# A gated linear attention with routed experts on one core: chunks laid out by halves, one product instruction a step of the running products, and a block closed without the drain of GpSimd's queue

## What is computed

```
mag = sqrt(a_re**2 + a_im**2); scale = min(mag, 0.999) / (mag + 1e-6)
a = (a_re + i a_im) * scale                        # complex gate, per batch, head, token, dim
for t in range(S):                                 # S = 768, B = 4, H = 8, D = 48
    state = a[t][:, None] * state                  # complex
    state.re += outer(k[t], v[t])
    y[t] = q[t] @ state.re
x = y as (B*S, H*D) = (3072, 384)
e = argmax(x @ w_gate + modality_bias[modality_id]); g = its softmax weight   # 8 experts
x = g * (relu(x @ w1[e]) @ w2[e])                  # w1 384x1024, w2 1024x384
out = ((x @ mid_w1) * (x @ mid_w2)) @ w3 @ w_out
```

## Time and profile before

| what | value |
|---|---|
| time, median of 3 runs | 917.78 us (916.23 to 918.56) |
| time of the profiled execution | 917.5 us, of which its span is 915.7 us |
| PE busy | 768.6 us (84%) |
| DVE busy | 496.7 us (54%) |
| ACT busy | 331.2 us (36%) |
| POOL busy | 128.7 us (14%) |

### The profile page before, as it was taken

How to read it: one execution, slowest core, us unless ns; L and a number is a source line. 1 busy time by engine, 2 the same in 40 slices (tenths; PEclk the granted TensorE clock), 3 DMA queues, 4 the chain that set the end, 5 groups by cost and what they waited for, 6 DMA issues and landing times.

```text
span 915.7 us, 11775 instructions
## 1 busy us (share of the span) xinstructions
PE 768.6 (84%) x4541; PEld 641.9 (70%) x4541; DVE 496.7 (54%) x963; ACT 331.2 (36%) x657; POOL 128.7 (14%) x127
## 2 busy tenths in 40 slices
PE   0029910399999999899999999999999999999995
PEld 0015500188888888787888888888989898988885
DVE  4999999999899975866453454341111111212010
ACT  6932100354545434534453452333122222223120
POOL 0201100000000032410000000013232222323231
PEclk9999965599999999999999999999999999999998
DMA  9982120456666656427423430160000000000000
GB/s 380 373 270 83 69 87 0 122 147 172 185 180 165 188 161 206 141 81 238 147 96 104 128 106 9 73 207 1 35 0 35 1 26 9 18 18 9 26 1 35
DMA packets 46756, 99.19 MB, mean 108 GB/s; under 512 B 11616, under 2 KB 29920, under 8 KB 44384
## 3 DMA queue, kind: packets, MB, share of 16 engines
q1 hardware_dynamic: 41056, 79.37, 28.3%
q0 software_dynamic: 5632, 18.94, 5.9%
HBM read 60.32 MB, written 18.94 MB: 87 GB/s over the span
## 4 chain that ended last, share of the span: by engine, by line
PE 69%; DVE 19%; DMA 3%; ACT 3%; issue 2%; SPq 2%; POOL 1%; DVEq 0%
PE moe_bank L557 17%; PE moe_bank L558 17%; PE moe_bank L559 17%; PE bank L1347 4%; DVE rows L1056 3%; DVE rows L1057 3%; PE bank L1381 3%; DVE gates L1059 2%; PE bank L1397 2%; PE bank L1313 2%; DVE gates L1032 2%; DVE gates L1060 2%; DMA gates<-a_im 1%; PE bank L1401 1%; PE bank L1353 1%
## 5 line engine op out<-in xcount | busy, mean ns | idle before, releaser
L1934 DVE TENSOR_TENSOR u_sb<-x_in,moe_bank 128x512 f32<-128x512 f32 x48 | 33.0, 688 | 229.1 <-PE moe_bank L559 229.1
L1772 POOL TENSOR_TENSOR hid_lo<-u_sb,hid_hi 128x512 fp32r<-128x512 f32 x48 | 62.4, 1299 | 357.9 <-ACT hid_hi L1829 357.9
L557 PE MATMUL moe_bank<-xT_hi,w_hi 128*128 128x512 f32 x264 | 104.8, 397 | 0.0
L558 PE MATMUL moe_bank<-xT_lo,w_hi 128*128 128x512 f32 x264 | 104.8, 397 | 0.0
L559 PE MATMUL moe_bank<-xT_hi,w_lo 128*128 128x512 f32 x264 | 104.0, 394 | 0.0
L1326 PE MATMUL bank<-early_w_out,early_w3T 128*128 128x384 f32 x128 | 45.4, 512 | 66.3 <-DMA early_w_out<-w_out 62.9
L1326 PEld LDWEIGHTS bank<-early_w_out,early_w3T 128*128 128x128 f32 x128 | 24.9, 199 | 86.3 <-issue 65.0
L1848 ACT COPY x_in<-moe_bank 128x512 f32<-128x512 f32 x48 | 28.1, 586 | 143.7 <-PE moe_bank L559 143.7
L559 PE MATMUL moe_bank<-w_hi,hid_lo 128*128 128x384 f32 x192 | 64.5, 336 | 0.0
L557 PE MATMUL moe_bank<-w_hi,hid_hi 128*128 128x384 f32 x192 | 64.4, 335 | 0.0
L558 PE MATMUL moe_bank<-w_lo,hid_hi 128*128 128x384 f32 x192 | 64.4, 335 | 0.0
(11 more groups left out here) (219 smaller groups left out, 1641.1 us busy)
## 6 DMA issues: line engine op xcount, KB each, us to landing
stage<-w SPq DMA_DIRECT2D x10, 1536.0 KB, 8.3
ks<-mags SPq DMA_DIRECT2D x48, 144.0 KB, 2.8
x_sorted<-early_zero POOLq DMA_DIRECT2D x8, 772.0 KB, 21.9
qs<-gates SPq DMA_DIRECT2D x40, 146.2 KB, 2.7
gates<-a_re SPq DMA_DIRECT2D x4, 1170.0 KB, 12.3
gates<-a_im SPq DMA_DIRECT2D x4, 1170.0 KB, 14.7
x_in<-x_sorted SPq DMA_DIRECT2D x24, 193.0 KB, 3.0
spare<-k SPq DMA_DIRECT2D x4, 1152.0 KB, 5.4
```

The lines of the kernel that those rows point to most:

```text
L557: nc.tensor.matmul(out, l_hi, r_hi, start=first, stop=False)
L558: nc.tensor.matmul(out, l_hi, r_lo, start=False, stop=False)
L1772: nc.gpsimd.tensor_tensor(hid_lo[:, f], u_sb[:, f % 2], hid_hi[:, f].bitcast(F32), ALU.subtract).then_inc(u_lo_ready, 1)
L1934: nc.vector.tensor_tensor(u_sb[:, f % 2], a_sb[:, f % 2], bank_b[f % 2][:, :], ALU.mult).then_inc(u_ready, 1)
```

## The change

1. The host lays chunks out in token order, each half followed by one word of padding (pitch 65): `by_step` goes, `spaced` pads halves. All access patterns follow (`halved`, `of_halves`, `chunk_of_q`), and so do the causal mask, the token numbers, v, modality_id and the read-back in `recurrence`, in which rows of a chunk were in step order.
2. The two product instructions of a step become one of 576 elements, both inputs broadcast. The elements of token u that an instruction touches in `gates` are now 144 single words, 260 bytes apart, instead of 72 pairs.
3. In `join`, steps 0 and 1 issue one instruction each instead of two.
4. `keep_busy` issues 6 matmuls instead of 8.
5. The block is opened with `no_gpsimd_drain=True`: at its end the other four engines drain and all meet at a barrier made of semaphores alone, and POOL's own drain instruction is left out.

The core of the diff:

```diff
         prods = L.rows0[:, :, :].rearrange("p c v -> p (c v)")[:, 0:4 * NG * BLK].rearrange(
-            "p (w c n h) -> p w c n h", w=2, c=2, h=2)
+            "p (w c n) -> p w c n", w=2, c=2)
...
-            return gates[:, x, b * GB:(b + 1) * GB].rearrange("p g (c t) -> p (g c) t", t=PITCH)[:, :, 0:CH]
+            return gates[:, x, b * GB:(b + 1) * GB].rearrange("p g (r t) -> p (g r) t", t=SUB + 1)[:, :, 0:SUB]
+
+        def halved(a):
+            return a.rearrange("p c (h t) -> p (c h) t", h=2)
...
-            at = gates[:, :, :, :].rearrange("p x g (c j h) -> p x (g c) j h", j=SUB + 1, h=2)
+            at = gates[:, :, :, :].rearrange("p x g (r j) -> p x (g r) j", j=SUB + 1)
+            both = [P, 2, 2, NG * BLK]
             for u in range(SUB - 1):
-                re, im = (at[:, x:x + 1, :, u].broadcast_to([P, 2, NG * NCH, 2]) for x in (RE, IM))
                 if u:
                     dve.wait_ge(prefix_step, u)
-                nc.vector.tensor_tensor(prods[:, 0], at[:, :, :, u + 1], re, ALU.mult)
-                nc.vector.tensor_tensor(prods[:, 1], at[:, :, :, u + 1], im, ALU.mult).then_inc(products, 1)
+                nc.vector.tensor_tensor(prods, at[:, :, :, u + 1].unsqueeze(1).broadcast_to(both),
+                                        at[:, :, :, u].unsqueeze(2).broadcast_to(both), ALU.mult).then_inc(products, 1)
...
-                    last = half[:, step, :, 0, SUB - 1:SUB].broadcast_to([P, part.stop - part.start, SUB])
+                    last = half[:, step:step + 1, :, 0, SUB - 1:SUB].broadcast_to([P, 2, part.stop - part.start, SUB])
                     out = (by_re, by_im)[step]
-                    for x in (RE, IM):
-                        ins = nc.vector.tensor_tensor(out[:, x], half[:, x, :, 1, 0:SUB], last, ALU.mult)
-                    ins.then_inc(halves_done, 1)
+                    nc.vector.tensor_tensor(out, half[:, :, :, 1, 0:SUB], last, ALU.mult).then_inc(halves_done, 1)
...
+            def chunk_of_q(m, i, c):
+                return qs[m][:, i, c * PITCH:(c + 1) * PITCH].rearrange("p (h t) -> p h t", h=2)[:, :, 0:SUB]
...
-            keep_busy(8, bank_scores[0])
+            keep_busy(6, bank_scores[0])
...
-        block = ctx.enter_context(nc.Block())
+        block = ctx.enter_context(nc.Block(no_gpsimd_drain=True))
```

More of the change, by code:

```diff
@@ L48, in constants @@
     put("ident", np.eye(P))
-    when = (row % 2) * SUB + row // 2
-    put("causal", (when[:, None] <= when[None, :]) * 1.0)
+    put("causal", (row[:, None] <= row[None, :]) * 1.0)
     put("before", (row[:, None] < row[None, :]) * 1.0)
@@ L64, in constants @@
     put("region", one * (n_tiles * CH * np.arange(n_experts)))
-    put("token", when[:, None] + CH * np.arange(n_tiles)[None, :])
+    put("token", row[:, None] + CH * np.arange(n_tiles)[None, :])
     put("step", one * np.arange(n_steps))
@@ L708, in plane, with of_halves @@
         def plane(x, b):
-            return gates[:, x, b * GB:(b + 1) * GB].rearrange("p g (c t) -> p (g c) t", t=PITCH)[:, :, 0:CH]
+            return gates[:, x, b * GB:(b + 1) * GB].rearrange("p g (r t) -> p (g r) t", t=SUB + 1)[:, :, 0:SUB]
+        def halved(a):
+            return a.rearrange("p c (h t) -> p (c h) t", h=2)
+        def of_halves(part):
+            return slice(2 * part.start, 2 * part.stop)
         first_part = -(-HU * D // P) * NCH
@@ L829, in re_square @@
                 act.wait_ge(gates_in[b][RE], landed(b))
-                nc.scalar.activation(mags[b][:, :, :], plane(RE, b), ACT.Square).then_inc(re_squared, 1)
+                nc.scalar.activation(halved(mags[b][:, :, :]), plane(RE, b), ACT.Square).then_inc(re_squared, 1)
             def im_square(b):
                 act.wait_ge(gates_in[b][IM], landed(b))
-                nc.scalar.activation(squares[b], plane(IM, b), ACT.Square).then_inc(im_squared, 1)
+                nc.scalar.activation(halved(squares[b]), plane(IM, b), ACT.Square).then_inc(im_squared, 1)
             def root(b):
@@ L877, in square @@
                 out = (norms[b], seeds[b])[x]
-                nc.scalar.activation(out[:, part], plane(x, b)[:, part], ACT.Square).then_inc(p_squared, 1)
+                nc.scalar.activation(halved(out[:, part]), plane(x, b)[:, of_halves(part)], ACT.Square).then_inc(p_squared, 1)
             def log(k):
@@ L1012, in im_square @@
                 dve.wait_ge(gates_in[b][IM], landed(b))
-                nc.vector.tensor_tensor(squares[b], plane(IM, b), plane(IM, b), ALU.mult).then_inc(im_squared, 1)
+                nc.vector.tensor_tensor(halved(squares[b]), plane(IM, b), plane(IM, b), ALU.mult).then_inc(im_squared, 1)
             def add(b):
@@ L1031, in scale @@
                 for x in (RE, IM):
-                    ins = nc.vector.scalar_tensor_tensor(out=plane(x, b), in0=mags[b][:, :, :], scalar=1.0, in1=plane(x, b),
+                    ins = nc.vector.scalar_tensor_tensor(out=plane(x, b), in0=halved(mags[b][:, :, :]), scalar=1.0, in1=plane(x, b),
                                                          op0=ALU.subtract, op1=ALU.mult, reverse0=True)
@@ L1066, in join @@
                 b, part = stages[k]
-                half = gates[:, :, b * GB:(b + 1) * GB].rearrange("p x g (c j h) -> p x (g c) h j", j=SUB + 1, h=2)[:, :, part]
+                half = gates[:, :, b * GB:(b + 1) * GB].rearrange("p x g (c h j) -> p x (g c) h j", j=SUB + 1, h=2)[:, :, part]
                 by_re = seeds[b][:, part].rearrange("p c (x j) -> p x c j", x=2)
@@ L1134, in early_q @@
                 for x in (RE, IM):
-                    out = L.early_q[:, x].rearrange("p g (c t) -> p (g c) t", t=PITCH)[:, :, 0:CH]
-                    nc.vector.tensor_tensor(out, plane(x, 0)[:, parts[0]], q_in[:, parts[0]], ALU.mult).then_inc(q_early_ready, 1)
+                    out = L.early_q[:, x].rearrange("p g (r t) -> p (g r) t", t=SUB + 1)[:, :, 0:SUB]
+                    nc.vector.tensor_tensor(out, plane(x, 0)[:, of_halves(parts[0])], halved(q_in[:, parts[0]]),
+                                            ALU.mult).then_inc(q_early_ready, 1)
             for step in range(3):
@@ L1346, in tensor @@
                     for i in range(HU):
-                        mm = nc.tensor.matmul(bank_scores[g % 2][:, i * CH:(i + 1) * CH], ks[m][:, i, c * CH:(c + 1) * CH],
-                                              qs[m][:, i, c * PITCH:c * PITCH + CH], start=True, stop=True)
+                        mm = nc.tensor.matmul(bank_scores[g % 2][:, i * CH:(i + 1) * CH].rearrange("p (h t) -> p h t", h=2), ks[m][:, i, c * CH:(c + 1) * CH],
+                                              chunk_of_q(m, i, c), start=True, stop=True)
                     mm.then_inc(scores_psum, 1)
@@ L1400, in tensor @@
                             for i, out, wide in zip(heads, outs, (HALF, D)):
-                                mm = nc.tensor.matmul(out, state[:, i * D:i * D + wide],
-                                                      qs[before % NU][:, i, last * PITCH:last * PITCH + CH], start=False, stop=True)
+                                mm = nc.tensor.matmul(out.rearrange("p (h t) -> p h t", h=2), state[:, i * D:i * D + wide],
+                                                      chunk_of_q(before % NU, i, last), start=False, stop=True)
                     mm.then_inc(yT_psum, 1)
@@ L1504, in sync @@
                     for h in range(2):
-                        sp.dma_start(L.rows(b)[h:P:2, :, 0:DM], io["x_rows"][b * S:(b + 1) * S, :].rearrange(
+                        sp.dma_start(L.rows(b)[h * SUB:(h + 1) * SUB, :, 0:DM], io["x_rows"][b * S:(b + 1) * S, :].rearrange(
                             "(c h j) v -> h j c v", h=2, j=SUB)[h]).then_inc(rows_back, DMA)
@@ L2113 @@
     arrays = {
-        "a_re": spaced(a_re), "a_im": spaced(a_im), "k": by_step(k), "q_packed": by_step(q), "q": by_dim(q),
-        "v": np.ascontiguousarray(v.transpose(0, 2, 1, 3).reshape(NT, 2, SUB, H * D).transpose(2, 1, 0, 3)
-                                  ).reshape(CH, NT, H * D),
+        "a_re": spaced(a_re), "a_im": spaced(a_im), "k": packed(k), "q_packed": packed(q), "q": by_dim(q),
+        "v": np.ascontiguousarray(v.transpose(0, 2, 1, 3).reshape(NT, CH, H * D).transpose(1, 0, 2)),
         "a_re_d": by_dim(a_re), "a_im_d": by_dim(a_im), "k_d": by_dim(k),
```

21 lines of the change are left out of this document (10 added, 11 removed).

## The result

The changed kernel takes 942.62 us (median of 4 runs, 942.03 to 944.32), against 917.0 for the kernel before in the same series. The ratio is 1.0279, with a 95% interval of 1.0261 to 1.0296. The sign, the place and the stated range held. The point, 964.5, was too high by 22 us: a loss of 47 us was forecast and 25.6 came, little more than half.

What follows compares the result with a forecast made beforehand. The prediction took DVE's running products and the chain behind them as the bound up to 212 us, then PE. 917.5 + 52.0 (single words) - 0.45 (join) - 4.5 (drain) = 964.5 us; range 929 to 971.

Steps and rivals of the forecast that it cites:

- The sign: Whole kernel: slower, given a chance of 0.81, against 0.17 for faster and 0.02 for the same.
- the place: The loss was to arise in the 63 steps of the running products on DVE, ahead of the first join.
- What bounds the kernel: DVE's running products and its chain to L1124, then SP's DMAs, then PE; DVE's delays up to 212 us move the end.
- Single words are slower: Running products on DVE: elements no longer in neighbouring pairs cost more than 1.04 ns each; 52.0 us lost.
- The rate, 2.08 ns: Running products on DVE: twice 1.04 ns for each single word, read or written; the 576-element product's elements take 1.20 us.
- The writes, 0.15 us for each of two instructions: Subtraction and addition of each step, L1064 and L1065: writing single words raises each from 0.31 to 0.46 us.
- the softer penalty: Rival for the running products: single words cost 1.66 to 1.8 ns; 930 to 949 us, chance 0.15.
- Slow reads, fast writes: Rival for the running products: only reads of single words are slow, 33.1 us lost; 945.6 us, chance 0.20.
- The drain, 4.5: End of the block: leaving out POOL's drain gains 4.5 us, three quarters of at most 6.1.
- The join, 0.45: Joins on DVE up to 212 us: six merged product pairs save 0.075 us each, 0.45 us gained.
- the matmuls on constants, 0: `keep_busy` on PE: two matmuls fewer gain nothing, hidden behind DMAs and DVE's joins; 1.6 us without this cover.
- Broken runs on PE: Scores and outputs read two runs of 64 words, costed at nothing; as a rival 7 us more, some 971.

Runs made afterwards that it cites:

- table of distances: `stride_table`, a kernel of its own timing mainly DVE instructions over words at various distances; 576 products took 758 ns contiguous, 1188 ns at 65 words.
- before_join_no_drain: The kernel before with the join's products merged in steps 0 and 1 and no drain at the block's end; 911.83 us, ratio to before 0.9952.
- after_two_products: The changed kernel with each step's product issued as two instructions of 288 elements again, over the same single words; 950.9 us, ratio to before 1.035.
- before_6_matmuls: The kernel before with 6 matmuls on constants for 8; 917.15 us against 916.93, ratio 1.0009.

## Why the prediction came out as it did

- **What bounds the kernel**: right, in the main. From 192.9 to 204.8 us the chain of the kernel before runs over ACT and PE, and not over DVE as the prediction has it up to L1124; but they had themselves begun late by DVE, so the lateness went through. The 32.5 us by which the first join is late are 32.3 late at SP's issues and 31.4 at the landing ahead of PE.
- **Single words are slower**: right, the step on which the sign rested. The small reductions had carried the true price, 1.7 to 1.8 ns. The Trainium skill, page Advanced Engine Details and Errata, section SBUF Cachelines, asks for two hits on a line of 16 bytes, and the table of distances agrees: no loss at 2 words, part of it at 3 and, but for the ups and downs further out, the full loss from 4. The Trainium skill's page VectorE: DVE Perf Modes, section Mode 1× (REGULAR), has weird strides work at one result a cycle; 1194 ns for 576 single words, against 758 for contiguous ones, say otherwise.
- **The rate, 2.08 ns**: the term that was mis-sized. By the table 144 contiguous elements take 308 ns and 576 take 758, so the fixed part of an instruction is 158 ns, and the measured rate is (1194 - 158) / 576 = 1.80 ns. I had three rows at 1.7 to 1.8 and rounded them to two clocks, because I took the regular pattern of the small ones for a relief. No row had shown such a relief. The product then spans 1.24 us from start to start and not 1.385, which is 0.145 x 63 = 9.1 us of the error.
- **The writes, 0.15 us for each of two instructions**: too much by half. Each lasts 0.11 us longer, and not 0.15, because the rate is softer here too. And the second starts while the first one's writes are still under way (0.26 after it, against 0.23), so only the lateness of the last is waited for. Both cost 0.15 together, and 0.30 - 0.15 = 0.15 is another 9.5 us of the error. The case whose mechanism came is the softer penalty, 1.8 ns both ways, at 949, which had a chance of 0.15; with this overlap it gives 917.5 + 63 x (1.24 + 0.26 + 0.45 - 1.425) - 4.95 = 945.6. *Slow reads, fast writes* has the same 945.6 in the prediction, and so is the nearest by its number, but that is luck: it left out the 0.15 us of the writes and had reads at 2.08 ns.
- **The drain, 4.5**: 5.4 by the runs, 6.0 by the distance from the last landing to the end. The row at the start of the program would have given 6.1; the quarter that I took off was for parts of the run-down that the traces don't show.
- **The join, 0.45, and the matmuls on constants, 0**: from the first join to SP's issues the kernel before takes 58.33 us and the changed one 58.11, so 0.2 is gained here and 0.3 in `before_join_no_drain`. The matmuls measured nothing beyond the spread. The prediction had the gap closed by the landing of the last DMA to `ks` and the clock's rise where it was. The rise came earlier, PE stood for 1.26 us, and the clock then fell; it cost 0.1 us at most, since DVE, the cover that the prediction names, just held.
- **Broken runs on PE**: nothing. At the high level the chain has the scores' 8 passes at 1.09 us in both kernels.

In sum: the step was forecast at 2.25 us and is 1.938 on average over the 63, 63 x 0.312 = 19.7 us (9.1 and 9.5 of it as above, the rest rounding); the drain gave 0.9 more. 964.5 - 19.7 - 0.9 = 943.9, against 942.6 measured. Of the remaining 1.3 us, 0.5 is that the sum began at 917.5 and the kernel before has 917.0 in this series; the rest is no more than the spread of the runs (942.0 to 944.3).

## What to carry to other kernels

Where a loop works on one time step of many sequences by TENSOR_TENSOR, lay two sequences alternately, so that every access of VectorE finds two neighbouring words: here that was worth 0.58 us a step (1.425 for the 2.00 of `after_two_products`), and the instruction saved 0.06 (1.94 for 2.00). Whether the pairs could be had together with one product instruction, no run here shows. Before an access pattern is changed, look in the trace for any instruction that already reads at such a distance, however small, and take its cost per element as it stands, best from the same kind of instruction. And look behind the last landing: a block that ends with GpSimd's DMAs can hide several microseconds there.

## What the runs showed of the hardware that I had not expected

- A distance of 64 words is worse than 65: 1442 ns against 1188 for the same 576 products, and 16 words are a little better than 8 (1122 against 1191). I have no explanation.
- Pairs that begin at word 3 of every 130 take 354 ns, those that begin at word 0 and 2 take 308: which words make up a pair matters. Counted from the tensor's start, the pairs at word 3 begin in turn 12 and 4 bytes behind a multiple of 16, so every other one lies across such a multiple, and the pairs at word 0 and 2 never do. That fits the price, but only these starts were tried.
- The price depends on the instruction: TENSOR_SCALAR pays 0.40 ns more an element over single words, TENSOR_TENSOR 0.80 (L93 and L95, L91 and L77 above). Why, no run shows.
- ScalarE and GpSimd pay as well, on 144 elements: ScalarE 311 ns contiguous (L108), 443 when it reads (L110) and 445 when it writes (L112) single words 65 apart; GpSimd 425 contiguous (L125) and 498 reading single words 65 apart (L127). Groups by form of `stride_table`:

```profile
L127 POOL TENSOR_TENSOR wide<-src 128x144 f32<-128x144 f32 x8 | 4.0, 498 | 0.6
L112 ACT COPY dst<-src 128x144 f32<-128x144 f32 x8 | 3.6, 445 | 0.3
L110 ACT COPY wide<-src 128x144 f32<-128x144 f32 x8 | 3.5, 443 | 0.3
L125 POOL TENSOR_TENSOR wide<-src 128x144 f32<-128x144 f32 x8 | 3.4, 425 | 171.0 <-ACT dst L112 170.4
...
L108 ACT COPY wide<-src 128x144 f32<-128x144 f32 x8 | 2.5, 311 | 158.7 <-DVE wide L95 158.5
```

- In the changed kernel the granted clock is at 1.00 while PE stands for 1.26 us (up to 215.54) and up to 217, and at 0.60 and 0.55 in the four microseconds after that, with PE busy throughout; behind the gap of 0.35 us in `before_6_matmuls` it stayed at 1.00.
